# A recurrence in 24 groups: parity pairs for the state transposes, an inverse transposed on VectorE, units of two and four groups, later loads of r, k and v

## The reference

```python
for t in range(S):
    y[:, :, t] = np.einsum('bhd,bhde->bhe', rt, state)
    Sa = np.einsum('bhde,bhe->bhd', state, at)
    state_decay = state * wt[:, :, None, :] - np.einsum('bhd,bhe->bhde', Sa, bt)
    state = state_decay + np.einsum('bhd,bhe->bhde', vt, kt)
...
h = x @ w_in;  g = 0 if h <= -1, (h + 1)**2 / 4 if |h| < 1, else h;  x = g @ w_out
h = max(x @ w1, x @ w2, x @ w3);  out = h @ w_last
```

## Time and profile before

| | |
|---|---|
| median of 3 runs | 1125.46 us |
| profiled execution | 1124.24 us |
| its span | 1122.5 us |
| recurrence, first xy done to last | 109 to 457 us |
| dense layers | 463 us to the end |
| PE / PEld busy | 990.3 us (88%) / 836.2 us (74%) |
| DVE / ACT / POOL busy | 458.4 / 397.7 / 417.5 us |
| mean granted TensorE clock | 0.96 |

### The profile page before, as it was taken

How to read it: one execution, slowest core, us unless ns; L and a number is a source line. 1 busy time by engine, 2 the same in 40 slices (tenths; PEclk the granted TensorE clock), 3 DMA queues, 4 the chain that set the end, 5 groups by cost and what they waited for, 6 DMA issues and landing times.

```text
span 1122.5 us, 33072 instructions
## 1 busy us (share of the span) xinstructions
PE 990.3 (88%) x13874; PEld 836.2 (74%) x13874; DVE 458.4 (41%) x620; ACT 397.7 (35%) x726; POOL 417.5 (37%) x609
## 2 busy tenths in 40 slices
PE   5628999899888988277799999999999999999998
PEld 4516887787777777256688878888887888788887
DVE  7724555454553221267533332333243333323331
ACT  1104454555444454244322332333133223323321
POOL 3284948476682820012312321332233123223311
PEclk9958999999999998789999999999999999999999
DMA  9715576665745341344200000000000000000000
GB/s 122 123 25 118 94 146 100 115 125 113 127 82 110 65 90 34 91 129 136 78 1 24 1 29 2 23 0 28 0 23 28 0 23 0 28 0 24 1 1 24
DMA packets 254736, 64.10 MB, mean 57 GB/s; under 512 B 235280, under 2 KB 250384, under 8 KB 254608
## 3 DMA queue, kind: packets, MB, share of 16 engines
q1 hardware_dynamic: 117328, 40.92, 15.9%
q10 hardware_dynamic: 137280, 21.32, 11.8%
HBM read 46.47 MB, written 15.73 MB: 55 GB/s over the span
## 4 chain that ended last, share of the span: by engine, by line
issue 25%; PE 18%; POOL 10%; DVE 3%; ACT 2%; DMA 1%; SPq 0%; POOLq 0%; DVEq 0%; ACTq 0%
POOL hid_lo L1232 10%; PE ring L1040 7%; PE acc L1040 5%; PE ring L1050 3%; PE ring L1082 1%; PE acc L1104 1%; DMA raw<-in_moe_w_dram 1%; ACT hid_hi L1165 1%; DVE clip L1289 1%; DVE sq L1295 0%; DMA x<-xT 0%; DVE wmax_lo L1258 0%; DVE win_lo L1258 0%; DMA raw<-in_moe_w_in_dram 0%; DVE wout_lo L1250 0%
## 5 line engine op out<-in xcount | busy, mean ns | idle before, releaser
L1232 POOL TENSOR_TENSOR hid_lo<-sq,hid_hi 128x512 fp32r<-128x512 f32 x132 | 170.0, 1288 | 487.6 <-ACT hid_hi L1165 487.6
L377 POOL TENSOR_TENSOR prod<-sysX 128x30 f32<-128x30 f32 (+9 forms) x180 | 93.1, 517 | 80.7 <-DMA sysX<-systems 68.6
L1194 ACT ACTIVATE sq<-clip 128x512 f32<-128x512 f32 x96 | 60.7, 633 | 170.7 <-DVE clip L1289 169.3
L1289 DVE TENSOR_SCALAR clip<-ring 128x512 f32<-128x512 f32 x96 | 66.2, 690 | 132.2 <-PE ring L1050 132.1
L1165 ACT CAST hid_hi<-sq 128x512 fp32r<-128x512 f32 x132 | 82.0, 621 | 83.0 <-DVE sq L1295 61.2
L381 POOL TENSOR_TENSOR sysX<-sysX,prod 128x30 f32<-128x30 f32 (+9 forms) x180 | 97.3, 540 | 14.1
L1040 PE MATMUL acc<-hid_hi,wout_hi 128*128 128x512 f32 x192 | 78.2, 407 | 21.0 <-POOL hid_lo L1232 21.0
L1040 PE MATMUL ring<-x_hi,win_hi 128*128 128x512 f32 x192 | 75.7, 394 | 18.1 <-DVE win_lo L1258 18.1
L1295 DVE SCALAR_TENSOR_TENSOR sq<-clip,sq 128x512 f32<-128x512 f32 x96 | 66.2, 690 | 57.0 <-ACT sq L1194 57.0
L1040 PE MATMUL acc<-hid_lo,wout_hi 128*128 128x512 f32 x192 | 76.3, 397 | 0.0
L1040 PE MATMUL acc<-hid_hi,wout_lo 128*128 128x512 f32 x192 | 76.2, 397 | 0.0
(11 more groups left out here) (159 smaller groups left out, 2240.7 us busy)
## 6 DMA issues: line engine op xcount, KB each, us to landing
xT<-yT SPq DMA_DIRECT2D x96, 40.0 KB
out_dram<-res SPq DMA_DIRECT2D x24, 160.0 KB, 1.8
nat_w<-in_w_dram ACTq DMA_DIRECT2D x44, 80.0 KB, 3.4
nat_a<-in_a_dram ACTq DMA_DIRECT2D x44, 80.0 KB, 3.6
nat_b<-in_b_dram ACTq DMA_DIRECT2D x44, 80.0 KB, 3.0
nat_r<-in_r_dram ACTq DMA_DIRECT2D x44, 80.0 KB, 3.1
nat_k<-in_k_dram ACTq DMA_DIRECT2D x44, 80.0 KB, 3.4
raw<-in_moe_w_out_dram SPq DMA_DIRECT2D x11, 320.0 KB, 3.1
```

Source lines behind the costliest of these rows:

```text
L377: g_.tensor_tensor(some, X[:, 0:j, j:j + 1].to_broadcast([P, j, rest]), X[:, j:j + 1, j + 1:BLK].to_broadcast([P, j, rest]), ALU.mult)\
L1194: nc.scalar.activation(sq[f % 2][:, :], clip[f % 2][:, :], ACT.Square, bias=0.5, scale=0.5).then_inc(squared, 1)
L1232: nc.gpsimd.tensor_tensor(hid[at % HB][1][:, :], sq[at % 2][:, :], f32(hid[at % HB][0][:, :]), ALU.subtract)\
L1289: nc.vector.tensor_scalar(clip[f % 2][:, :], ring[(f + 2) % 4][:, :], -1.0, None, ALU.max).then_inc(clipped, 1)
```

## The change

**State transposes by parity.** `vrv` and `zrz` hold their heads as (parity, pair); r is loaded by parity. `st` makes four 128x128 transposes, which put the state of batches and pairs into other halves, and `ys` runs in two turns over all four combinations of halves, the second turn behind a wait for the first. `rv` and `rz` use a new function for the new order of heads. The loads of r and v are split by parity, so each has four DMAs per group instead of two.

**Inverse transposed on DVE.** `inv` is no longer stored and loaded: one DVE transpose per group (L737 of the changed kernel) makes it from `invT`. `solX`, the ACT copy, its store and two of six loads per group are gone.

**Units.** There are seven instead of six: groups 0-1, 2-5, 6-9, 10-13, 14-17, 18-21, 22-23. POOL may begin a unit three turns before its first group at position 4 of its list, formerly four turns before at position 7.

**Loads.** The start loads of r, k, v stand behind the load of the first unit in SP's queue; the later loads of r and v move from ACT to SP. **Tables.** All `ORDER`, `START` and `BANK` entries are new, and DVE's masks are made behind its first `a`.

```diff
+UNITS = [(0, 2), (2, 4), (6, 4), (10, 4), (14, 4), (18, 4), (22, 2)]
-            "POOL": [("step", 0), ("step", 0), ("step", 0), ("stTc", -1), ("kn", 2), ("step", 0), ("step", 0),
-                     ("total", -1), ("step", 0), ("step", 0), ("step", 0), ("step", 0), ("step", 0), ("step", 0),
+            "POOL": [("step", 0), ("step", 0), ("step", 0), ("step", 0), ("step", 0), ("step", 0), ("step", 0),
+                     ("step", 0), ("step", 0), ("step", 0), ("total", -1), ("step", 0), ("step", 0), ("step", 0),
+                     ("kn", 2), ("stTc", -1)],
-            "SP": [("solved", 0), ("inverse", 0), ("system", 7), ("unit", 7), ("y", -1)],
+            "SP": [("solved", 0), ("load r0", 2), ("load v0", 2), ("inverse", 0), ("system", 7), ("load r1", 3),
+                   ("unit", 7), ("load v1", 3), ("y", -1)],
-        FIRST_STEP = {0: 0, 1: 73}
-        SOLVE_FROM, SOLVE_AT = 4, 7
+        FIRST_STEP = {0: 0, 1: 48}
+        SOLVE_FROM, SOLVE_AT = 3, 4
@@ load
+                if n in ("r", "v"):
+                    for s in range(2):
+                        eng.dma_start(by_parity(n, g, j)[:, s], src.rearrange("(p s) t e -> s t p e", s=2)[s])\
+                            .then_inc(loaded[n][g % NATS[n]], 16)
@@ SP
-            for g in range(4):
-                for n in ("r", "k", "v"):
-                    if g < NATS[n]:
-                        for j in range(2):
-                            load(sp, n, j, 0)(g)
@@ load_unit
+                if u == 0:
+                    for at in range(4):
+                        for n in ("k", "r", "v"):
+                            if at < NATS[n]:
+                                for j in range(2):
+                                    load(sp, n, j, 0)(at)
@@ store_unit
-                sp.wait_ge(solX_made[u % 2], u // 2 + 1)
-                sp.dma_start(xd[u % 2].rearrange("i j h m t -> (i j h) (m t)"),
-                             solX[:, :, :].rearrange("r m t -> r (m t)"))\
-                    .then_inc(x_stored[u % 2], 16)
@@ inverse
-                    sp.dma_start(inv[g % 2][j * CH:j * CH + BLK, :, :],
-                                 xd[u % 2, i, j].rearrange("h t m -> t h m")).then_inc(inv_loaded[g % 6], 16)
@@ DVE
+            def inverse(g):
+                dve.wait_ge(inv_loaded[g % 6], 16 * 4 * (g // 6 + 1))
+                ...
+                ge(dve, done["p"], g - 1)
+                nc.vector.transpose(inv[g % 2][:, :, :], invT[g % 3][:, :, 0:BLK]).then_inc(inverted, 1)
@@ PE
+            def scores_by_parity(ps, lhs, rhs):
+                for s in range(2):
+                    for q in range(HP // 2):
+                        for j in range(2):
+                            for i in range(2):
+                                at = (2 * s + q) * CH
+                                last = nc.tensor.matmul(ps[rows(j), i, at:at + CH],
+                                                        lhs[rows(i), 2 * s + q, j, :], rhs[rows(i), 2 * s + q, j, :],
@@ st
-                    for p in range(HP):
-                        for s in range(2):
-                            at = (j * HP + p) * W
-                            last = nc.tensor.matmul(ps[rows(s), 0, at:at + W], stT[g % 2][rows(s), j, p, :],
+                    for q in range(HP // 2):
+                        at = (2 * j + q) * P
+                        last = nc.tensor.transpose(ps[:, 0, at:at + P],
+                                                   stT[g % 2][:, j, 2 * q:2 * q + 2, :].rearrange("r i d -> r (i d)"),
@@ ys
+                for turn in range(2):
+                    if turn == 1:
+                        pe.wait_ge(done["ys"], 2 * g + 1)
+                    for q in range(HP // 2):
+                        for i in range(2):
+                            for s in range(2):
+                                p, j = 2 * q + i, i ^ turn
+                                last = nc.tensor.matmul(ps[rows(s), j, p * P + CH:(p + 1) * P],
+                                                        st[g % 2][rows(i), j, q, s, :],
+                                                        rT[g % LATE][rows(i), 2 * s + q, j, :],
```

More of the change, by code:

```diff
@@ L142, in attention @@
         diag_set = [sem(f"diag_set{i}") for i in range(2)]
-        solX_made = [sem(f"solX_made{i}") for i in range(2)]
         x_stored = [sem(f"x_stored{i}") for i in range(2)]
@@ L151, in attention @@
         CLEARED = EARLY + LATE + NATS["r"] + NATS["v"] + 2
-        ZEROED = len(invT) + len(stT) + len(st) + 1
+        ZEROED = len(invT) + len(stT) + len(st) + 2
         SOLVE = 2 * (BLK - 2)
@@ L169, in sequence, with up_to, stored_systems, loaded_systems @@
                         yield n, s + ahead
+        unit_of = {g: u for u, (first, many) in enumerate(UNITS) for g in range(first, first + many)}
+        def up_to(u, each):
+            return sum(each(many) for v, (_, many) in enumerate(UNITS) if v <= u and v % 2 == u % 2)
+        def stored_systems(u):
+            return up_to(u, lambda many: 16 * 4 * many)
+        def loaded_systems(u):
+            return up_to(u, lambda many: 16 * (1 if many == UNIT else 2))
         def program(eng, steps):
@@ new lines, in load_unit @@
+                ge(sp, x_stored[u % 2], 16 * (u // 2))
+                if u == 0:
+                    sp.wait_ge(zeroed, ZEROED)
+                if many == UNIT:
+                    sp.dma_start(sysX[u % 2][:, :, :].rearrange("r m t -> r (m t)"),
+                                 sysd[u % 2].rearrange("q i j h m t -> (q i j h) (m t)"))\
+                        .then_inc(sys_loaded[u % 2], 16)
+                else:
+                    for q in range(2):
+                        sp.dma_start(sysX[u % 2][rows(q, many * 2 * H), :, :].rearrange("r m t -> r (m t)"),
+                                     sysd[u % 2, q, 0:many].rearrange("i j h m t -> (i j h) (m t)"))\
+                            .then_inc(sys_loaded[u % 2], 16)
@@ L313, in store @@
                         sp.dma_start(dst, yT[rows(s, D), j, :, :]).then_inc(y_stored, 16)
-            program("SP", {"system": system, "unit": load_unit, "solved": store_unit, "inverse": inverse, "y": store})
+            program("SP", {"system": system, "unit": load_unit, "solved": store_unit, "inverse": inverse, "y": store}
+                    | {f"load {n}{j}": load(sp, n, j, NATS[n]) for n in ("r", "v") for j in range(2)})
             sp.wait_ge(y_stored, 64 * NG)
@@ L333, in _ @@
                 g_.memset(x, 0.0).then_inc(cleared, 1)
-            for x in stT + invT + st + [total]:
+            for x in [sysX[0]] + stT + invT + st + [total]:
                 g_.memset(x[:], 0.0).then_inc(zeroed, 1)
@@ L552, in ys @@
                 ps = begin("ys", g)
-                for p in range(HP):
-                    for j in range(2):
-                        for s in range(2):
-                            last = nc.tensor.matmul(ps[rows(s), j, p * P + CH:(p + 1) * P],
-                                                    st[g % 2][rows(s), j, p, :], rT[g % LATE][rows(s), p, j, :],
-                                                    start=p == 0, stop=False, skip_group_check=True)
-                last.then_inc(done["ys"], 1)
+                for turn in range(2):
[8 more added lines that the diff above has]
+                                                        rT[g % LATE][rows(i), 2 * s + q, j, :],
+                                                        start=turn == 0 and q == 0, stop=False, skip_group_check=True)
+                    last.then_inc(done["ys"], 1)
             def xy(g):
@@ L763, in y_ @@
                     .then_inc(out["y"], 1)
-            program("DVE", {"scan": scan, "dn": dn, "bn": scale(dve, nc.vector, "b", bn, EARLY, bn_made), "a": a_,
+            program("DVE", {"inverse": inverse, "scan": scan, "dn": dn, "bn": scale(dve, nc.vector, "b", bn, EARLY, bn_made), "a": a_,
                             "n": n_, "ak": ak_, "rv": rv_, "rz": rz_, "x": x_, "y": y_})
```

142 lines of the change are left out of this document (71 added, 71 removed), and 28 rows, old and new, of tables (ORDER, START).

## The result

The changed kernel takes 1110.19 us (median of 4 runs, 1105.3 to 1113.59), the kernel before, on the same chip, 1125.42 (4 runs, 1123.57 to 1126.03): ratio 0.9864, 95% interval 0.9825 to 0.9903. The forecast of 1107.7 us in 1086 to 1120 held. The profiled execution took 1110.72 us, its span 1109.0, 13.5 us less than the span of before.

The account below looks back on a forecast made before the run. PE was taken to bound the steady recurrence, a POOL and memory chain the start. Stages -14.7, pauses -1.3, start -2.5 and clock +2 gave -16.5 us from 1124.2: 1107.7 us, range 1086 to 1120.

Parts of the forecast that it names:

- part 4: Start, a chain through POOL and memory: first p 14 us earlier, second unit's wait gives back 11.5, net -2.5 us; clock +2.
- (a): Start: n of group 1 leaves DVE at 27.6, POOL's first step 9.25 us later at 36.9, 11.9 earlier.
- (b): Start: POOL's steps and diagonal still take 36.8 us, plus one kn of 0.84, ending at 74.5.
- (c): Start: store, invT issues, landing, transpose and hand-overs take 8.7 us; first p at 83.2 instead of 97.23.
- (d): Start: POOL solves unit 1 only after unit 0, so p of group 2 waits until 123.4.
- (e): Start: PE's clock is low after the wait for unit 1, costing 0 to 3.3 us, taken as +2.
- Part 1: PE's stages: st -0.34, ys -0.63, wait between ys turns +0.2, tile sizes +0.1: -0.67 us per group, times 22 groups.
- rival "more": New tables remove PE's pauses and waits, or unit 1 doesn't bind: another 16 us, about 1091; chance 0.22.
- Part 3: Work moved between engines: ACT's relief gains no time, DVE's 0.6 us transpose and SP's 20 issues (9.7 us) are covered.
- Part 2: PE's pauses inside stages: 12 of some 244 products per group go, 0.06 us per group, 22 x 0.06 = -1.3 us.
- Part 5: Later units, begun three turns ahead: solved in time with 3.8 us of slack, no cost.
- slower rival: PE waits for late inverses at p of groups 6, 10, 14, 18, 22: 1128 if 8 us late; chance 0.10.

Follow-up runs that it names:

- e_units3: Changed kernel with units of 3, 4, 4, 4, 4, 4 and 1 groups: 1109.34 us, ratio 0.9883 to the kernel before.
- e_units4: Changed kernel with six units of four groups, no short first unit: 1110.72 us, ratio 0.9885 to the kernel before.
- e_nopair: Changed kernel with the old layout of r, v, z and st and the old st and ys: 1118.12 us, ratio 0.9961 to the kernel before.
- e_same: The changed kernel itself, run again as a base: 1109.4 us, ratio 0.9858 to the kernel before.
- e_ysplit: Changed kernel with rz run between the two turns of ys: 1110.93 us, ratio 0.9846 to the kernel before.
- e_b_loads_sp: Kernel before, with the whole loop loads of r and v issued by SP instead of ACT: 1118.85 us, ratio 0.9987.
- e_pair_only: Kernel before with pairing by parity alone, its r and v loads by half their heads on ACT: 1136.11 us, ratio 1.0066.
- e_loads_act: Changed kernel with the loop loads of r and v back on ACT: 1193.17 us, ratio 1.0572 to the kernel before.
- e_twice: Changed kernel with each DVE transpose of the inverse done twice: 1103.96 us, ratio 0.986 to the kernel before.
- e_r_act: Changed kernel with only r's loop loads back on ACT: 1129.13 us, ratio 1.0083 to the kernel before.

## Why the prediction was right, point by point

**The start (part 4)** was right in its mechanism and nearly in its numbers. (a) n of group 1 left DVE at 26.08 (27.6 forecast) and the first step began 7.71 us later, at 33.79 (36.9): the hand-over through memory was 1.5 us shorter. (b) The solve with its kn took 39.0 us (37.6). (c) From there to the first p, 83.64 - 72.83 = 10.8 us (8.7). The 28 first loads took 0.71 us each and not 0.48, but they were issued by 51.5 and weren't in the way. The store went out at once (72.86), and the last of the four loads was issued at 78.05; the transpose stood behind other work in DVE's order, without a wait of its own:

```profile
76.00 2.05 SPq L330 DMA_DIRECT2D invT<-inverses_T  x4
```
```profile
81.61 0.67 DVE L772 TENSOR_TENSOR nT<-pair,neg 128x512 f32<-128x512 f32 x1
82.20 0.45 DVE L737 STREAM_TRANSPOSE inv<-invT 128x256 f32<-128x256 f32 x1
```

The errors cancel, which is luck: 83.64 for 83.2. (d) p of group 2 at 122.69 for 123.4, after 7.94 us on DVE's transpose. e_units3 and e_units4 show that this is the unit's chain: with three or four groups in the first unit no p at the start waits. (e) The low clock lasted from 122.69 to 128.4, 5.7 us at half speed, 2.9 lost where I took 2.

**Part 1, PE's stages**: the mechanism is shown (e_nopair), the term was mis-sized in two ways. PE's busy time fell by 0.88 us a group (0.72 against e_same's profile), about as the sum has it without the turn wait (0.34 + 0.63 - 0.1 = 0.87). The turn wait was too small: inside ys it comes to 0.37 us (0.83 - 0.46) and not 0.2, of which e_ysplit could give back little. Then st and ys gain 0.34 + 0.26 = 0.60, less 0.1 for the tile sizes: 0.5, as the profile of e_nopair has it. And "x 22" was wrong: in the last eight groups PE is not the bound (11.5 us busy of 13.5 before, 10.9 of 13.2 after), and pairing gives nothing there. 13 x 0.5 is 6.5 us, not 14.7; over whole executions e_nopair says 8.7 (medians) to 11.6 us (ratios, 1.03%), still less than 14.7.

**What I had not in the sum** filled the gap, and that the total came within 3 us of the forecast is luck to this extent. The steady groups gained 0.92 us each, some 0.4 more than pairing gives; e_nopair has 0.35 of them (15.71 for 16.06), 0.24 of it less idle time, which is the mechanism of the rival "more" at a third of its size. That profile flatters e_nopair, as said, so the 0.35 may be less. Of its 4 us in all the runs don't say how much is order and how much the loads on SP: e_b_loads_sp leaves anything from 0 to 0.4%.

**Part 3** failed as reasoning, though its zero wasn't far off. I wrote that ACT loses four issues at "no gain in time, since PE, not ACT, is the bound", and read ACT's 124 us of 250 in the earlier trace rows as idle capacity. The busy time of that view leaves DMA issues out. With them ACT was nearly full, and the layout by parity needs 16 issues where the loads were: e_pair_only is 0.66% slower than before, e_loads_act 5.7%. So the move to SP is no extra of this change: in the old orders it takes away what pairing loses, and in the new ones the places tried for them on ACT were bad. Whether there is a good one was not tried. I also left out that a PE that waits more can run on a lower clock (0.95 and 0.83 in those two). SP's 20 issues I priced at 9.7 us of 15; SP's queue waits only 16.6 us in 195, so they fill about nine tenths of it. DVE's transpose took 0.45 us (0.6 guessed) and is covered: e_twice.

**Part 2, pauses** (0.06 us a group): idle time per group went from 1.63 to 1.69 us with 6% fewer matmul records, but that includes the new turn wait. The part with no releaser went from 1.26 to 1.13, and lies between 0.88 (e_units3) and 1.62 (e_ysplit) in kernels with the same products. So no run here can tell the term of 0.06 from nothing. By the Trainium skill's rule (Runtime: NRT & Kernel Launch, Instruction fetch mechanics) it was nothing; the traces don't contradict that. What pauses PE inside a stage stays open.

**Part 5** held nearly: in the steady part no p waits for an inverse. Two do in the last eight, where the groups are 13 us long: group 17's for 2.45 us and group 18's, the first of a unit, for 1.81.

```profile
352.80 0.69 PE L522 MATMUL single<-inv,nT 32*32 32x32 f32 x32 [2.45 <-DVE inv L737]
...
366.62 0.70 PE L522 MATMUL single<-inv,nT 32*32 32x32 f32 x32 [1.81 <-DVE inv L737]
```

The slower rival's mechanism shows at that one place; one such wait of 1.59 us stood in the last eight before. Behind these waits the granted clock falls as well: over the last eight groups it is 0.89, against 0.92 before.

**The way to the dense layers** was no term, and cost 2.6 us. From the flag `unsafe` on DVE to the first load of x on SP it takes 3.5 us in the kernel before, 6.2 in the changed one (449.93 - 443.70):

```profile
443.70 0.14 DVE L824 TENSOR_SCALAR unsafe<-pair 1x1 int32<-1x1 f32 x1 [0.78 <-PE pair L630]
...
449.93 2.59 SPq L1064 DMA_DIRECT2D x<-xT  x4
```

In e_twice, which differs by 24 instructions of DVE alone, it is 4.0 us:

```profile
439.55 0.15 DVE L826 TENSOR_SCALAR unsafe<-pair 1x1 int32<-1x1 f32 x1 [0.77 <-PE pair L631]
...
443.55 2.59 SPq L1066 DMA_DIRECT2D x<-xT  x4
```

SP's longer stream isn't the cause: e_b_loads_sp has it and takes 3.5 us. In the fourteen profiles the time goes with the number of DVE's instructions: 3.5 to 4.0 us in the four kernels with 620, 5.8 to 6.5 in the nine with 644, 4.0 in e_twice with 668. Whether that is the cause, and how, these runs don't show.

No kernel tried here beats the changed one by more than the intervals allow.

## What to carry to other kernels

Before calling an engine idle, add its DMA issues to its busy time: they are work of that engine (0.6 us each on ACT here), and four of them in a row ahead of a copy delayed that copy by all four. A wait of PE can cost more than its length: look at the granted clock of the stretch, too (0.83 where PE waited most). A layout that cuts transfers into more pieces is paid for on the issuing engine; look for who has room, and for another transfer to drop. And multiply a gain per turn only by the turns in which the engine is the bound.

## What had not been expected of the hardware

- A DMA issue by ACT mostly took 0.60 to 0.65 us whether it moved 80 KB or 40 KB. On SP four issues of 40 KB in a row took 2.6 to 4.0 us (r at 32.82 and 39.50 us).
- A wait of TensorE for its own stage just issued: ys, with one between its turns, took 0.37 us more than rz, with as many products and no such wait (0.83 for 0.46); 0.32 in the earlier trace rows.
- The vector engine's transpose of 128x256 in 32x32 blocks took 0.45 us, a little less than its 128x320 sum `xsum` (0.48).
- With twenty-four more instructions in one engine's stream a hand-over between blocks was 2 us shorter (e_twice, one profile).
- Where TensorE waited more, its granted clock was lower: 1.00 over the steady part of the changed kernel (1.69 us idle of 15.14 a group), 0.92 in e_r_act (2.5 of 16.7), 0.83 in e_loads_act (4.9 of 20.1).
